# Softmax reciprocals taken once on 32 rows and half the columns, then written to all rows by DMA, in a fused attention, MLP and soft-MoE kernel

## The reference

```
q_pool = q.reshape(B, H, S // 2, 2, D).mean(axis=3)      # B=4, H=8, S=1152, D=64
scores = scale * q_pool @ k^T ; scores -= max over keys ; attn = exp(scores)
attn = attn / (sum over keys + 1e-09)
x = attn @ v                                             # 576 queries per head
h = x @ w_in ; g = where(h > 0, h, exp(min(h, 0)) - 1) ; x = g @ w_out   # 2304 tokens, 512 -> 2048 -> 512
logits = x @ phi ; soft MoE with 8 experts of 4 slots each, dispatch and combine
```

## Time and profile before

| what | value |
|---|---|
| median of 3 runs | 932.74 us (932.3 to 933.03) |
| the profiled execution | 933.13 us, of which the span of the trace is 931.1 us |
| mean granted TensorE clock | 0.996 |
| PE busy | 901.1 us, 97% of the span |
| DVE busy | 568.9 us, 61% |
| ACT busy | 387.7 us, 42% |
| POOL busy | 389.2 us, 42% |

### The profile page before, as it was taken

How to read it: one execution, slowest core, us unless ns; L and a number is a source line. 1 busy time by engine, 2 the same in 40 slices (tenths; PEclk the granted TensorE clock), 3 DMA queues, 4 the chain that set the end, 5 groups by cost and what they waited for, 6 DMA issues and landing times.

```text
span 931.1 us, 17697 instructions
## 1 busy us (share of the span) xinstructions
PE 901.1 (97%) x7120; PEld 728.4 (78%) x7120; DVE 568.9 (61%) x966; ACT 387.7 (42%) x740; POOL 389.2 (42%) x269
## 2 busy tenths in 40 slices
PE   4899999999999999999999999999999999999996
PEld 3676766677676766665999999999999999999733
DVE  6988888888888988866554433433443433433423
ACT  3555555565555555555443222322322322322202
POOL 3999999999999989988000000000000000000000
PEclk9999999999999999999999999999999999999999
DMA  6112212222212212303320000200000000377898
GB/s 240 46 59 77 71 36 74 78 78 77 73 57 77 62 43 77 95 1 114 91 91 1 1 1 1 91 1 1 1 1 1 1 1 1 122 239 225 286 382 307
DMA packets 47025, 76.39 MB, mean 82 GB/s; under 512 B 3296, under 2 KB 32608, under 8 KB 46944
## 3 DMA queue, kind: packets, MB, share of 16 engines
q1 hardware_dynamic: 46944, 75.26, 24.2%
HBM read 70.53 MB, written 4.72 MB: 81 GB/s over the span
## 4 chain that ended last, share of the span: by engine, by line
PE 88%; DVE 5%; POOL 2%; DMA 2%; SPq 1%; issue 1%; ACT 1%; POOLq 0%; ACTq 0%
PE psum L611 14%; PE psum L680 8%; PE psum L682 7%; PE psum L664 7%; PE psum L662 7%; PE psum L681 7%; PE psum L663 7%; PE psum L590 6%; PE psum L533 4%; PE psum L593 3%; PE psum L595 3%; PE psum L597 3%; DVE mx L1142 2%; POOL acc L1499 2%; PE psum L493 1%; SPq L469 1%
## 5 line engine op out<-in xcount | busy, mean ns | idle before, releaser
L1499 POOL TENSOR_TENSOR acc<-acc,pt 128x576 f32<-128x576 f32 x220 | 324.1, 1473 | 33.8 <-ACT pt L936 2.8
L936 ACT ACTIVATE pt<-psum 128x576 f32<-128x576 f32 x288 | 174.1, 649 | 121.7 <-PE psum L598 120.6
L1142 DVE TENSOR_REDUCE mx<-psum 128x1 f32<-128x512 f32 x256 | 162.0, 676 | 25.9 <-PE psum L533 25.1
L611 PE MATMUL psum<-pt,vs 128*64 128x288 f32 x1152 | 154.9, 414 | 0.0
L1330 DVE TENSOR_SCALAR gf<-gf 128x384 f32<-128x384 f32 x96 | 34.5, 359 | 196.4 <-ACT gf L1065 196.4
L680 PE MATMUL psum<-gh,W 128*128 128x384 f32 x384 | 133.4, 347 | 0.0
L1065 ACT ACTIVATE gf<-psum 128x384 f32<-128x384 f32 x96 | 47.2, 492 | 200.8 <-PE psum L664 200.2
L681 PE MATMUL psum<-gl,W 128*128 128x384 f32 x384 | 128.5, 335 | 0.0
L682 PE MATMUL psum<-gh,W 128*128 128x384 f32 x384 | 128.4, 334 | 0.0
L664 PE MATMUL psum<-xh,W 128*128 128x384 f32 x384 | 128.4, 334 | 0.0
L662 PE MATMUL psum<-xh,W 128*128 128x384 f32 x384 | 128.4, 334 | 0.0
(11 more groups left out here) (163 smaller groups left out, 1835.5 us busy)
## 6 DMA issues: line engine op xcount, KB each, us to landing
ring<-in_w SPq DMA_DIRECT2D x16, 1024.0 KB, 5.2
ring<-in_w SPq DMA_DIRECT2D x32, 512.0 KB, 7.8
qraw<-in_qT SPq DMA_DIRECT2D x16, 576.0 KB, 4.8
kraw<-in_kT SPq DMA_DIRECT2D x16, 576.0 KB, 3.7
vs<-in_v SPq DMA_DIRECT2D x16, 576.0 KB, 4.0
out<-ob SPq DMA_DIRECT2D x18, 256.0 KB, 4.4
wst<-in_w_in SPq DMA_DIRECT2D x16, 256.0 KB, 2.7
wst<-in_w_out SPq DMA_DIRECT2D x16, 256.0 KB, 3.0
```

What stands on the lines that cost most here:

```text
L611: ins = mm(psum[64 * s:64 * s + 64, O_BANK, 0:HALF], vs[:, p % NB, s, kt * D:(kt + 1) * D], pt[:, i % NPT, s, :], start=(kt == 0), stop=(k ...
L936: act.activation(pt[:, i % NPT, :, :], t_pair(("T", h, kt))[:, :, 0:HALF], ACT.Exp, scale=SCALE)\
L1142: dve.tensor_reduce(mx[:, b, u // 2, s, u % 2:u % 2 + 1], bank, AX.X, ALU.max).then_inc(s_red, 1)
L1499: pool.tensor_tensor(a, first, pt[:, i % NPT, :, :], ALU.add).then_inc(s_acc, 1)
```

## The change

PE still makes the sums of a step in one PSUM bank, but only 144 columns wide: in the first 32 rows of each head it puts the sums of the first 144 queries, in the other 32 rows those of the last 144. For this `ones` becomes 96 columns wide, zeros, ones, zeros, and the product is taken with two shifted pieces of it. ACT copies 128x144 into a new tile `rc`, DVE takes one reciprocal of 128x144, and SP writes the result with eight small DMAs (32 rows of 144 values each) into `rinv`, where every row again holds all 288 values. The rest of SP's queue is put in another order around these DMAs.

```
-    ones = sb("ones", [P, 64])
+    ones = sb("ones", [P, 96])
...
+        ("rc", [P, HALF // 2], F32))
...
-        for p in range(NP):
-            if p + 3 < NP:
-                load_q(p + 3)
-                load_k(p + 3)
-            if p + 3 < NP:
-                load_v(p + 3)
-        sp.wait_ge(s_qs, NP)
-        for f in range(NF):
+        def spread_reciprocals(h):
+            sp.wait_ge(s_rec, h + 1)
+            if h:
+                sp.wait_ge(s_o, h)
+            for s in range(2):
+                for k in range(2):
+                    for to in range(2):
+                        sp.dma_start(rinv[64 * s + 32 * to:64 * s + 32 * to + 32, k * (HALF // 2):(k + 1) * (HALF // 2)],
+                                     rc[64 * s + 32 * k:64 * s + 32 * k + 32, :]).then_inc(d_rinv, 16)
+        def load_weights(f):
...
+        for p in range(NP):
+            if p == NP - 1:
+                for f in range(NST):
+                    load_weights(f)
+            if p:
+                spread_reciprocals(2 * p - 1)
+                if p + 2 < NP:
+                    load_v(p + 2)
+            if p == NP - 1:
+                for f in range(NST, NST + W_EARLY):
+                    load_weights(f)
+            spread_reciprocals(2 * p)
+            if p + 3 < NP:
+                load_q(p + 3)
+                load_k(p + 3)
+        for f in range(NST + W_EARLY, NF):
+            load_weights(f)
+        spread_reciprocals(NH - 1)
...
-            for s in range(2):
-                ins = mm(o[64 * s:64 * s + 64, 0:HALF], ones[:, :], acc[:, h % 2, s, :], start=True, stop=(by_pool == KT - 1))
-            for kt in range(by_pool + 1, KT):
-                for s in range(2):
-                    ins = mm(o[64 * s:64 * s + 64, 0:HALF], ones[:, :], pt[:, (KT * h + kt) % NPT, s, :],
-                             start=False, stop=(kt == KT - 1))
+            parts = [acc[:, h % 2, :, :]] + [pt[:, (KT * h + kt) % NPT, :, :] for kt in range(by_pool + 1, KT)]
+            for k in range(2):
+                rows, some = ones[:, 32 - 32 * k:96 - 32 * k], slice(k * (HALF // 2), (k + 1) * (HALF // 2))
+                for n, part in enumerate(parts):
+                    for s in range(2):
+                        ins = mm(o[64 * s:64 * s + 64, 0:HALF // 2], rows, part[:, s, some], start=(k == 0 and n == 0),
+                                 stop=(k == 1 and n == len(parts) - 1))
...
             if h:
-                act.wait_ge(s_o, h)
+                act.wait_ge(d_rinv, 128 * h)
-            act.copy(rinv[:, :], bank[:, 0:HALF]).then_inc(s_sum, 1)
+            act.copy(rc[:, :], bank[:, 0:HALF // 2]).then_inc(s_sum, 1)
...
-        def reciprocals(h, part):
+        def reciprocals(h):
             dve.wait_ge(s_sum, h + 1)
-            some = rinv[:, part * (HALF // 2):(part + 1) * (HALF // 2)]
-            dve.reciprocal(some, some).then_inc(s_rec, 1)
+            dve.reciprocal(rc[:, :], rc[:, :]).then_inc(s_rec, 1)
         def normalize(h):
-            dve.wait_ge(s_rec, 2 * (h + 1))
+            dve.wait_ge(d_rinv, 128 * (h + 1))
...
-                if h and kt == 7:
-                    reciprocals(h - 1, 1)
```

More of the change, by code:

```diff
@@ L94, in soft_moe_kernel @@
                           ("qlr", [P, NB, SQ], F32R))
-    (_, kraw, qs, nmT, pt, vs, acc, khr, qhr, bdq, onesel, nm2, mx, rinv, qraw) = overlay(
+    (_, kraw, qs, nmT, pt, vs, acc, khr, qhr, bdq, onesel, nm2, mx, rinv, qraw, rc) = overlay(
         ("early_weights", [P, W_EARLY * 4 * 512], F32),
@@ L109, in soft_moe_kernel @@
         ("rinv", [P, HALF], F32),
-        ("qraw", [P, 2, SQ], F32))
+        ("qraw", [P, 2, SQ], F32),
+        ("rc", [P, HALF // 2], F32))
     NG, NST = 3, 3
@@ L152, in soft_moe_kernel @@
     d_eye, d_sel, d_add4, d_phi = sems("d_eye d_sel d_add4 d_phi")
-    d_q = sem("d_q")
+    d_q, d_rinv = sem("d_q"), sem("d_rinv")
     d_k = [sem(f"d_k{i}") for i in range(NB)]
@@ L617, in _ @@
         first_max_rows()
-        pe.wait_ge(s_one, 2)
+        pe.wait_ge(s_one, 3)
         for h in range(NH):
@@ L1119, in _ @@
     def _(dve):
-        dve.memset(ones[:, :], 1.0).then_inc(s_one, 1)
+        dve.memset(ones[:, :], 0.0).then_inc(s_one, 1)
+        dve.wait_ge(s_one, 1)
+        dve.memset(ones[:, 32:64], 1.0).then_inc(s_one, 1)
         dve.memset(psum[:, Y_BANKS[3], :], 0.0).then_inc(s_one, 1)
@@ L1230, in _ @@
                     if h:
-                        reciprocals(h - 1, 0)
+                        reciprocals(h - 1)
                 reduce_items(s_items(h, kt))
@@ L1335, in _ @@
                     weights_lo(f + WLEAD)
-                if c == 0 and f in (11, 13):
-                    reciprocals(NH - 1, (f - 11) // 2)
+                if c == 0 and f == 11:
+                    reciprocals(NH - 1)
                 if c == 0 and f == 14:
```

## The result

| | before | after |
|---|---|---|
| median | 932.88 us (932.3 to 933.1, 4 runs) | 1075.68 us (1072.82 to 1079.12, 4 runs) |
| span of the profiled execution | 931.1 us | 1070.9 us |
| mean granted clock | 0.996 | 0.946 |

The changed kernel is slower by a factor of 1.153 (95% interval 1.151 to 1.154), 143 us. The forecast had the side and the place right and half of the size.

What follows compares the result with a forecast made beforehand. PE was taken to bound the attention, any standstill paid in full. From 933.1 us, 48 for the late query load, 22 for PE's clock and 3 for PE's sums gave 1006 us, with a range of 958 to 1035 us.

Steps and rivals of the forecast that it cites:

- What bounds the kernel: In the attention PE sets the pace and pays any standstill in full; DVE has about 7.8 us of room in four steps.
- the 18.0 us of the earlier trace: Whole attention: PE's 35 waits for DVE to read unit scores, taken as the most a lighter DVE could give back.
- the 0.44 us of the earlier trace: PE's wait at each turn into an odd step, behind the removed reciprocal; 14 turns to give up to 6 us.
- `normalize`: Odd steps: its wait for the copies costs 0 to 0.4 us, paid for by the missing reciprocal; booked at 0.
- the faster rival: E, about 920 us: queries come in time and PE regains most of its 18.0 us of waits; chance 0.03.
- The moved query load: Turns into even steps: queries queued behind eight copies land late, PE stands 3.7 us, 13 times, 48 us.
- the bound of 4.1 us: Upper bound for SP issuing the eight copies: 8 x 0.51 us, the `w_out` median; 3.0 us was taken.
- The landing of 4.0 us: Time from the query load's issue to its data landing, taken between 3.6 (minimum) and 4.8 us (median).
- PE's clock: After each of 13 stops the clock falls to half for 3.4 us, costing 1.7 us: 22 us, bounds 0 and 44.
- PE's sums: Two matmuls of 288 columns become four of 144: 0.1 us a step, 3 us over 32 steps, at most 13.
- The rest booked at nothing: ACT's copy and wait, first weights issued at step 29, last copies of steps 30 and 31, memset of `ones`: 0.
- the case where both are dear (1045): Rival D: issues 0.5 us, landing 4.8; 71 us stall, 22 clock, 14 `normalize`, 3 sums; chance 0.08.

Runs made afterwards that it cites:

- e4: The kernel before, with a step's second reciprocal cut to 2 of 144 columns and products using the first 96 queries' reciprocals, no copies: 933.1 us, 1.000.
- e1: The changed kernel with the query load back right behind the v load, ahead of the even step's reciprocal copies: 977.9 us, 1.048 of before.
- e5: The changed kernel with two copies of 128 rows instead of eight of 32, same bytes, crossing of the halves left out: 970.5 us, 1.039.
- e3: The changed kernel with 24 unread matmuls ahead of PE's wait at kt 2 of even steps: 1057.7 us, 1.133 of before.
- e8: e1 with normalize moved in DVE's program from kt 0 to kt 3 of a step: 954.0 us, 1.022.
- e9: The kernel before with the tile of ones 96 columns wide instead of 64, shifting later tiles by 128 bytes: 938.1 us, 1.004.
- e12: The kernel before with ones declared last and 128 bytes of padding in its place: 937.4 us, 1.005.
- e11: e8 with the first five MLP weights earlier in SP's queue and ones (96 wide) declared behind the other tiles: 942.8 us, 1.010.

## Why the prediction was right and wrong

*What bounds the kernel:* right that PE's time in the attention is paid in full, 137.9 us of stops and slow clock for 135.4 us of delay. Wrong about how near DVE was: I read the 18.0 us of the earlier trace rows as stops of PE and the 0.44 us of the earlier trace rows as time to be had. They are mostly the weight loader's. `e4` shows a gain of 0. In my sum it was set against `normalize`, and it gave the faster rival a prize that did not exist.

*The moved query load:* the mechanism held link by link (`e1`, `e5`). The term was 48 us, 13 x 3.7; the 13 stops are 5.7 us apiece in the mean, 73.9 us. **The step that failed is the price of an issue.** I took "the lowest, 0.33, and 0.04 between two, 3.0 us for eight"; measured are 0.51 for the first, 0.59 for each that follows, and 0.04 between, 5.0 us. The 0.33 us belongs to `kraw`, a load from HBM that was issued alone, and it misled in two ways. The kind counts most: a copy inside SBUF takes 0.51 us even with nothing ahead of it, and no row of the trace before had one. The place in the queue adds some 0.1 us, and rows for that were there: the query load takes 0.47 us behind the v load. Even the bound of 4.1 us, made from the dearest median of another kind, was too low. The landing of 4.0 us was right, 4.0 in the median.

*PE's clock:* right that it falls after these stops, and that rows at one event could price it in kind; `e3` shows that the loss is real. The term was 22 us and is 38. Two things were mis-sized. Behind the 13 stops the clock is low for 6.8 us, not 3.4, my upper bound; part of that passes while PE still stands, and 2.3 us are lost apiece instead of 1.7, 29.6 us. And the clock also falls behind six stops of 1.4 to 2.0 us, which I had not priced at all: 10.2 us. The Trainium skill, "TensorE: Matmul & The Clock Gate", section on HAM oscillation, which warns of a fall in every round of a loop that waits for DMAs, is borne out here: the clock falls at each of the 13 stops, and it is below 1.00 in each of the nine stretches of 53 us from 40 us to 517 us.

*`normalize`:* booked at 0 because "0.4 us that the missing reciprocal gives at the same turn pays for it". Nothing was given, and with issues of 0.63 us the copies land 6.3 us behind the reciprocal instead of 5: a stop of 1.2 us in the pair shown. I had written "if an issue takes 0.5 us the loss is 1 us, 14 us in all"; in the changed kernel the 14 stops at kt 4 of odd steps are 19.9 us, and `e8` measures 23.9 us for this wait in both kinds of steps, once the query load no longer hides the even ones. The 2.0 us of fixed cost in the Trainium skill, "DMA: Bandwidth & Descriptors", are given in its section "Anatomy of one DMA" for DMAs issued from GpSimd; here SP issues them, and the landing of 1.8 us in the median comes near. The sum with it failed by the issues ahead.

*PE's sums:* booked at 3 us, measured 0. Eight rows of 144 columns take 0.66 us, as four of 288 did.

*The rest booked at nothing:* the end of the attention was not nothing. In `e1` the MLP starts 15 us later than 25.4 us of lost steps explain. The runs behind it find 5.6 us in the weights; 6.0 us are two stops of PE in `e1` for which `normalize` had waited for its copies, and the rest is not taken apart. The tile that grew by 128 bytes was not in my list at all, and the MLP and what follows were 4.4 us longer, not "as long as before".

So the sum was 73 us and the loss 143. Of the 70 us between them the 13 stops make 26, the clock 16, the other stops of the attention, booked at 0, another 26, and what follows the attention 4; the 3 us booked for PE's sums come off. The range ended at 1035 because the price of an issue enters the stall and `normalize` together, and I let the case where both are dear (1045) fall outside. Even that case was not dear enough: its stall was 5.5 us and its clock 22.

## What to carry to other kernels

Before splitting a transfer into small DMAs, multiply their number by the time of an issue of that kind that stands right behind another, and see what is queued behind them: here eight copies of 18 KB cost 5 us of queue, while two with the same bytes cost 1.1. If the trace has no DMA of that kind, its cheapest row is no estimate for it. When work is taken off an engine, look first whether the bounding engine's own rows wait for it; waits on the weight loader's rows, or idle time of the engine itself, prove nothing, and a run that merely leaves the work out tells it in one go. When one unknown price enters several terms, carry it through all of them at once at both ends, or the range will be too short.

## What the runs showed of the hardware

- The issue of a copy inside SBUF holds SP for 0.51 us when nothing is ahead of it and 0.59 us behind another one, where a load of keys from HBM takes 0.33 us alone (`kraw` before). With 128 rows and four times the bytes it is 0.47 and 0.60 us (`e5`). The query load right behind the eight took 0.58 us, behind a v load 0.47.
- A copy of 18 KB inside SBUF lands 1.8 us after its issue (1.7 to 3.0); in `e5`, with 72 KB, 2.0 us (1.9 to 3.4).
- PE's granted clock fell to 0.50 behind stops as short as 1.25 us (before, at 417.9 us) and 1.4 us (changed kernel, at 362.0 us), and stayed at 1.00 behind others of 1.6 us (at 212.95 and 503.38 us).
- 128 bytes in the place of tiles changed the landing of 512 KB loads from 7.8 to 8.5 us (`e9`) and 8.7 us (`e12`), and the kernel by 4.5 us; with 256 bytes they landed in 7.7 us (`e11`).
- Matmuls that nobody reads, put into PE's long stops, made the kernel 18 us faster: the clock's loss fell from 39.7 to 13.3 us (`e3`).
